# A three-layer attention and mixer kernel: the rounded copy of the keys is made by GpSimd instead of ScalarE

## The reference

```python
scores = scale * np.matmul(q, k.transpose(0, 1, 3, 2))
keep = is_sink | in_window            # keys 0..3, or 0 <= query - key < 128
scores = np.where(keep, scores, -1e9)
a = softmax(scores)
x = a @ v                             # then heads side by side: 768 x 512 per batch
# layer 2
h = relu(x @ w_in); u, v = h[..., :512], h[..., 512:]
v_n = (v - mean(v)) / sqrt(var(v) + 1e-6)
x = (u * (w_spatial @ v_n + b_spatial)) @ w_out
# layer 3
u = x + (relu(x^T @ w_tok1) @ w_tok2)^T
out = u + relu(u @ w_ch1) @ w_ch2
```

## Time and profile before

| | |
|---|---|
| median of 3 runs | 519.94 us (519.16 to 520.16) |
| profiled execution, its own time | 519.94 us |
| its span | 518.2 us |
| PE busy | 497.9 us (96%) |
| DVE busy | 214.0 us (41%) |
| ACT busy | 161.3 us (31%) |
| POOL busy | 161.2 us (31%) |

### The profile page before, as it was taken

The page is one execution under the profiler, slowest core; times in us unless marked ns, Lnnn a source line. Parts: engine busy times, 40 slices in busy tenths (PEclk is TensorE's granted clock), DMA queues, the critical chain, the costliest instruction groups (busy, mean ns, idle before and its releaser), DMA issues.

```text
span 518.2 us, 7223 instructions
## 1 busy us (share of the span) xinstructions
PE 497.9 (96%) x2712; PEld 442.6 (85%) x2712; DVE 214.0 (41%) x535; ACT 161.3 (31%) x337; POOL 161.2 (31%) x170
## 2 busy tenths in 40 slices
PE   1799999999999999999999999999999999999997
PEld 1698899999999989999888999888888888888885
DVE  4577777687567326755222233112121121211212
ACT  2466666577566332112211232101101001011010
POOL 5365535453332377801307903940000000000000
PEclk9999999999999999999999999999999999999999
DMA  7444233433320134300202410400011000010002
GB/s 263 127 144 140 90 100 103 135 102 104 103 64 1 54 117 135 99 0 1 76 1 78 128 39 20 140 24 2 0 43 39 0 1 0 31 52 1 0 1 81
DMA packets 19479, 34.19 MB, mean 66 GB/s; under 512 B 2288, under 2 KB 4848, under 8 KB 19440
## 3 DMA queue, kind: packets, MB, share of 16 engines
q1 hardware_dynamic: 19008, 33.55, 20.6%
q10 hardware_dynamic: 432, 0.13, 0.1%
HBM read 30.53 MB, written 3.15 MB: 65 GB/s over the span
## 4 chain that ended last, share of the span: by engine, by line
PE 92%; DVE 3%; issue 1%; DMA 1%; ACT 1%; DVEq 0%; ACTq 0%
PE bank L933 25%; PE bank L934 24%; PE bank L935 24%; PE bank L1006 7%; PE bank L972 3%; PE bank L948 3%; PE bank L949 2%; PE bank L1014 1%; DVE q_st L751 1%; PE bank L988 1%; DMA mask_scratch<-key 1%; PE bank L1166 1%; PE bank L1164 1%; DVE masked L760 1%; PE bank L980 0%
## 5 line engine op out<-in xcount | busy, mean ns | idle before, releaser
L922 DVE SCALAR_TENSOR_TENSOR hch_lo<-bank,hch_hi 128x512 fp32r<-128x512 f32 x36 | 24.9, 692 | 153.8 <-ACT hch_hi L696 153.8
L696 ACT ACTIVATE hch_hi<-bank 128x512 fp32r<-128x512 f32 x36 | 21.5, 598 | 169.0 <-PE bank L935 169.0
L586 ACT ACTIVATE probs<-masked,small 128x288 f32<-128x288 f32 (+1 forms) x96 | 48.9, 509 | 51.3 <-DVE small L760 50.8
L495 POOL TENSOR_TENSOR k_lo<-k_raw,k_hi 128x512 fp32r<-128x512 f32 x24 | 30.9, 1287 | 85.0 <-ACT k_hi L561 85.0
L760 DVE CUSTOM_DVE_ANT_0 masked<-bank,masks 128x288 f32<-128x288 f32 (+1 forms) x96 | 41.0, 427 | 36.9 <-PE bank L949 32.0
L935 PE MATMUL bank<-up_hi,wc_lo 128*128 128x512 f32 x144 | 56.0, 389 | 0.0
L934 PE MATMUL bank<-up_lo,wc_hi 128*128 128x512 f32 x144 | 56.0, 389 | 0.0
L933 PE MATMUL bank<-hch_hi,wc_hi 128*128 128x512 f32 x144 | 56.0, 389 | 0.0
L934 PE MATMUL bank<-hch_lo,wc_hi 128*128 128x512 f32 x144 | 56.0, 389 | 0.0
L933 PE MATMUL bank<-up_hi,wc_hi 128*128 128x512 f32 x144 | 56.0, 389 | 0.0
L935 PE MATMUL bank<-hch_hi,wc_lo 128*128 128x512 f32 x144 | 56.0, 389 | 0.0
(11 more groups left out here) (119 smaller groups left out, 1052.1 us busy)
## 6 DMA issues: line engine op xcount, KB each, us to landing
k_raw<-kT SPq DMA_DIRECT2D x24, 256.0 KB, 3.0
q_raw<-qT SPq DMA_DIRECT2D x24, 256.0 KB, 3.0
stage<-w_c SPq DMA_DIRECT2D x24, 256.0 KB, 2.7
v_sl<-vL SPq DMA_DIRECT2D x12, 264.0 KB, 3.1
outT<-out_sb SPq DMA_DIRECT2D x12, 256.0 KB, 2.1
stage<-w_sp SPq DMA_DIRECT2D x12, 192.0 KB, 2.6
stage<-w_in SPq DMA_DIRECT2D x8, 256.0 KB, 4.4
stage<-w_out SPq DMA_DIRECT2D x4, 256.0 KB, 3.0
```

What stands on the lines that cost most here:

```text
L495: pool.tensor_tensor(k_lo[:, hs, c0:c0 + P], raw, k_hi[:, hs, c0:c0 + P], ALU.subtract).then_inc(k_ready, 1)
L586: act.activation(probs[:, n % N_PROB, 0:w], masked[:, n % N_MASKED, 0:w], ACT.Exp, bias=least[:, n % 8:n % 8 + 1], scale=-1.0).then_inc(ex ...
L696: act.activation(hch_hi[:, u[2] % N_HCH, :], bank[:, :], ACT.Relu).then_inc(hi_ready, 1)
L922: dve.scalar_tensor_tensor(out=hch_lo[:, f % N_HCH, :], in0=bank[:, :], scalar=0.0, in1=hch_hi[:, f % N_HCH, :], op0=ALU.max, op1=ALU.subt ...
```

## The change

The rounding copy of the keys for groups 2 to 23 is removed from ACT and put on POOL, in front of the subtraction, with the same two waits. For groups 0 and 1 it stays on ACT. The function `k_high` is cut to those two groups, and the loop of ACT no longer calls it.

```diff
@@ gpsimd, k_prepare(g)
                 raw = k_raw[:, g % 2, :].rearrange("p (h c) -> p h c", c=P)
+                if g >= 2:
+                    pool.wait_ge(s_k[g % 2], 16 * (g // 2 + 1))
+                    if g >= 4:
+                        pool.wait_ge(scored, 4 * (g - 1))
+                    pool.tensor_scalar(k_hi[:, hs, c0:c0 + P], raw, 1.0, 1.0, ALU.mult, ALU.mult).then_inc(k_high_done, 1)
                 pool.wait_ge(k_high_done, g + 1)
                 pool.tensor_tensor(k_lo[:, hs, c0:c0 + P], raw, k_hi[:, hs, c0:c0 + P], ALU.subtract).then_inc(k_ready, 1)
@@ scalar, k_high(g)
-                t, half = divmod(g, 2)
-                c0 = 0 if t % 2 == 0 else P + SINKS
-                act.wait_ge(s_k[g % 2], 16 * (g // 2 + 1))
-                if g >= 4:
-                    act.wait_ge(scored, 4 * (g - 1))
-                act.activation(k_hi[:, 4 * half:4 * half + 4, c0:c0 + P], k_raw[:, g % 2, :].rearrange("p (h c) -> p h c", c=P),
+                half = g % 2
+                act.wait_ge(s_k[g % 2], 16)
+                act.activation(k_hi[:, 4 * half:4 * half + 4, 0:P], k_raw[:, g % 2, :].rearrange("p (h c) -> p h c", c=P),
                                ACT.Copy).then_inc(k_high_done, 1)
@@ scalar, loop over the steps
-                if n % 4 == 0 and 2 <= n // 4 + 1 < N_GROUP:
-                    k_high(n // 4 + 1)
```

## The result

The changed kernel takes 522.99 us (median of 6 runs, 521.07 to 524.14), the one before 519.75 us beside it (6 runs, 518.87 to 520.16). The ratio is 1.0063, with the interval 1.0042 to 1.0085: slower, by about as much as predicted. The profiled execution took 523.14 us, its span 521.4 us, 3.2 us more than before.

A forecast was written before the change was run, and what follows sets the result against it. Until about 59 us `q_low` on DVE repeatedly holds PE; then to 191 us PE alone bounds. The profiled 519.94 us plus 1.1 (start) plus 1.75 (groups 4, 6, 8) gives 522.8 us, range 519.5 to 524.3.

The forecast's parts named there:

- How `q_low` and POOL take turns: Shared port of DVE and POOL: `q_low` stands still until the running POOL operation ends, then needs 0.55 us.
- The one row on which I chose the side: At 99.58 us, POOL began 0.02 us ahead of `q_low` and went first; so POOL was assumed first.
- Step 1: Start: group 2's and 3's `k_lo` delay `q_low` of groups 1 and 2; costs 1.1 us, bounds 0 to 2.4.
- Step 2: Groups 4, 6 and 8: `k_lo` starts 0.02 us before `q_low`, delaying it 1.06, 0.61 and 0.08; sum 1.75 us.
- `q_low` first: Rival: `q_low` precedes `k_lo` at groups 4, 6, 8; group 8 gains 0.52 us, total 520.5; chance 0.25.
- Step 3: Later groups: `q_low` falls into `k_hi`, PE has slack 0.6; priced 0, upper end 1 us, including normalisation at line 803.
- my own signs: Trace signs of being wrong: those three `q_low` take 0.69, the chain meets `k_lo` itself, or the difference arises behind 60 us.
- hidden: Rival: whole kernel, everything hidden since the chain is PE alone for most of the span; 519.9 us, chance 0.12.
- paid back: Rival: at the start, a later start loses only half of step 1; 522.2 us, no separate chance given.
- Not slower: Rival: ACT's copy at 16.58 goes, neither early `q_low` is caught, group 8 gains 0.52; 519.0 us, chance 0.08.

The follow-up runs named there:

- experiment 7: Experiment 2 plus a tiny DVE memset right before `q_low` of groups 6 and 8; 521.19 us, ratio 1.0034 to the kernel before.
- experiment 10: The changed kernel with the copy on POOL only from group 3 on, group 2 staying on ACT; 519.95 us, ratio 0.9997 to the kernel before.
- experiment 3: The changed kernel with the copy on POOL for groups 2 and 3 only; 522.95 us, ratio 1.0072 to the kernel before.
- experiment 9: The changed kernel with SP's transfers from its loop turn 4 on held until DVE has masked group 2's first score; 521.74 us, ratio 1.0036.
- experiment 11: Experiment 2 plus two one-column DVE operations before `q_low` of groups 6 and 8; 520.79 us, ratio 1.0020 to the kernel before.
- experiment 6: Experiment 2 with the copy done twice on POOL from group 6 on; 518.48 us, ratio 0.9983 to the kernel before.
- experiment 2: The changed kernel with the copy on POOL only from group 4 on, groups 2 and 3 staying on ACT; 518.64 us, ratio 0.9985.
- experiment 1: The changed kernel with POOL's copy, from group 2 on, held until `q_low` of the group before is done; 519.92 us, ratio 1.0006.
- experiment 5: Experiment 2 with POOL's copy held until `q_low` of the group before is done; 518.07 us, ratio 0.9974 to the kernel before.
- experiment 12: Experiment 10 with POOL waiting, from group 4 on, for `q_low` of the group before; 517.17 us, ratio 0.9956 to the kernel before.
- experiment 8: Experiment 7's memsets plus experiment 5's wait for `q_low` from group 4 on; 518.06 us, ratio 0.9973 to the kernel before.
- experiment 4: The changed kernel with POOL held behind `q_low` before the keys of groups 5, 7 and 9 only; 521.89 us, ratio 1.0045.

## Why the prediction held, step by step

**How `q_low` and POOL take turns** held in every trace: in the first 170 us of all fourteen profiled executions, every `q_low` that took over 0.85 us ends 0.53 to 0.56 us behind the end of a POOL operation. The one row on which I chose the side has a lead of 0.02 us, and at that lead POOL won again (group 4 of the changed kernel). But at groups 6 and 8 the leads were 0.01 us or less, and there nothing follows from it: with 0.01 POOL won at 6 of experiment 7 and at 4 and 8 of experiment 10, and DVE at 8 of the changed kernel and of experiment 7. It is a tie.

**Step 1 was mis-sized: 1.1 us predicted, 2.5 measured at group 3, or 3.3 without the head start.** `q_low` of group 1 took the predicted 1.35. The mask subtraction of line 734 was caught (1.39 for 0.29, +1.10), which I had in the upper bound of 2.4 and not in the sum. That makes 1.8 us; with the head start of 0.8, which is luck, group 2 started 1.04 late. `q_low` of group 2 ended at 20.02 against my 20.15, but that is luck too: I had it in a `k_lo`, with over 1.4 us, and it came behind that `k_lo`, met a `win_hi` and took 0.93. After that two things that I had not foreseen: the three mask operations of line 708 in the chain at 20 us, held by a `win_lo`, 0.67 longer, and the gap, 0.80 longer. 1.04 + 0.67 + 0.80 = 2.51. Experiments 3 and 10 show that group 2's copy makes all of this, experiment 9 the gap's part of it.

**Step 2 was right at one group of three: 1.75 predicted, 1.23 measured.** Group 4 took 1.80 and cost 1.06 and a little. At 6 and 8 the rival came true: `q_low` first, 0.69, nothing lost. Where POOL does win there, my price holds: in experiment 11 groups 6 and 8 lose 0.76 us against the kernel before (groups 4 to 9), and I had 0.61 + 0.08.

**What `q_low` first is worth was priced too low: 0.52 in the rival, 1.04 measured.** The changed kernel gains 0.47 at group 7, 0.30 at 8 and 0.27 at 9. I had seen 8 only. At 7 PE before had waited for `p_cat` of ACT. The waits of PE (us in total, times, longest), before and after, 27 to 72 us:

```profile
PE bank L980 <- ACT p_cat L594: 0.6, 1, 0.6
```
```profile
PE bank L980 <- ACT p_cat L596: 0.2, 1, 0.2
```

ACT's lost copy isn't the reason, since before it stood behind that `p_cat`:

```profile
47.81 0.30 ACT L594 ACTIVATE p_cat<-probs 128x128 f32<-128x128 f32 x1
48.01 0.62 ACT L561 ACTIVATE k_hi<-k_raw 128x512 fp32r<-128x512 f32 x1
```

It is `q_low` of group 6, which leaves DVE 0.5 us earlier when it isn't caught; the masking behind it, the exponential and `p_cat` come earlier by as much. Three experiments show it: in 6, 7 and 11 ACT is as relieved as in experiment 2, but `q_low` of group 6 takes 1.15, 1.81 and 1.71, and their gain at group 7 is 0.0, where experiment 2, with 0.69, gains 0.5. So the prediction was right that ACT's copy stands on no path to PE there, and wrong in following `q_low` to the next score only.

**Step 3 was priced at 0 and cost 0.66 us.** `q_low` behaved as I worked out (about 0.98 at later even groups, with PE not waiting for it). The normalisation did not: behind the later `q_low`, line 803 started at 75.62 beside a `k_lo` and took 1.00 us, and PE then waited 0.42 us for the next `p_cat` of ACT. That lies inside my bound of 1 us, and experiments 1 and 5 lose nothing there.

**The sum came out right since the errors cancel.** Predicted +1.1 +1.75 +0 = +2.9. The trace: +2.51 +1.23 -1.07 +0.66 -0.1 = +3.2. The closeness is luck: the head start of 0.8 and the gains at groups 7 to 9 hide the start's true cost. By my own signs the account was half right: two of the three `q_low` took 0.69, which I had named as a sign of being wrong, and 0.66 us arose behind 60 us, where the chain was to be PE alone. The sign of the change is shown by experiments 2, 3 and 10: what is lost is lost through whom POOL meets, not through how long it works (experiment 6). The rivals "hidden" and "paid back" fall. "`q_low` first" was half true. "Not slower" needed the first catch to fail, and experiments 2, 5 and 12 are that case.

**What stays open.** Why one side wins a tie of 0.01 us in one execution and the other in the next; that this makes the wide scatter of the changed kernel (3.1 us) and of experiment 10 (3.4), against 1.5 in experiment 12, is argued and not shown. The first load has its part in such scatter (1.3 us between the profiled executions), and so has the moment at which PE changes its pace (up to 0.9 us, last section). Both also stand in the differences between experiments: of the 2.8 us by which experiment 12 is ahead of the kernel before at group 11, 0.6 is there at group 0 and 0.9 arises between groups 3 and 4, of which `q_low`'s 0.69 instead of 0.74 explains nothing. And the kernel before had caught `q_low` of its own (1.19 and 1.72 at groups 6 and 8). No run gives it the wait without moving the copy, so how much of the gain of experiments 5 and 12 is the wait alone isn't known.

## What to carry to other kernels

When work goes to an engine that takes turns with another, as POOL and DVE do here, don't add up its length; list who runs on the other engine at the moment it starts, above all short operations on the path to PE, and see who is first. Where both are released by the same event and arrive within 0.01 us, don't predict the winner but fix it with a wait: here the same move is +0.6% as it stands and -0.4% with one wait and without its first group. Follow a DVE operation that ends earlier or later beyond the matmul that waits for it: here it fed ACT, and ACT fed the next matmuls. And a start that is full of waits is its own case: what frees a buffer earlier also starts a transfer earlier, in front of something else.

## What was not expected of the hardware

- DVE operations with one input are held too. Line 803 takes 0.54 us alone and 1.00 at 75.62, where it ends 0.28 us behind `k_lo`; at 181.43 it ended 0.27 behind a POOL subtraction. The prediction had this for line 803 but not for the masks of line 708, which took 1.20 for 0.53, three together. The Trainium skill says that it can happen (SBUF — State Buffer, Who interferes with whom): `tensor_scalar` can enter a mode that uses both ports and then contends. The durations here agree; no run shows which mode these operations were in.
- The gap in the chain at 20 to 26 us was 2.86 us before, where the instruction packets went ahead of the data, 2.79 in experiment 9, where transfers were held back, and 3.66 in the changed kernel, where they went behind. That the wait for them makes the gap fits experiment 9; no run took the fetch itself away.
- PE works at half its later pace until about 30 us, though the granted clock reads 1.00 in both stretches. In experiment 12 the start to start distance of 288-column scores falls from 0.24 to 0.13 us between 27.6 and 30.4 us (about 288 columns at 1.2 GHz and at 2.4), and eight matmuls of one kind take 1.00 us:

```profile
27.57 0.44 PE L955 MATMUL bank<-k_hi,q_st 128*128 128x288 f32 x1
27.81 0.44 PE L956 MATMUL bank<-k_lo,q_st 128*128 128x288 f32 x1
...
28.76 1.00 PE L1013 MATMUL bank<-v_sl,p_t 128*128 128x66 f32 x8
...
30.30 0.29 PE L955 MATMUL bank<-k_hi,q_st 128*128 128x288 f32 x1
30.43 0.29 PE L956 MATMUL bank<-k_lo,q_st 128*128 128x288 f32 x1
```

In the kernel before the eight took 1.74 us, at about the same place:

```profile
29.55 1.74 PE L1006 MATMUL bank<-v_sl,p_t 128*128 128x66 f32 x8
```

From the first score of group 3 to the transposes of x (line 988) PE takes 3.5 to 3.6 us in the two kernels and in experiments 2, 3, 7, 10 and 11, 3.4 in 1, 2.8 to 3.1 in 5, 6, 8 and 9, and 2.7 in 4 and 12. I have no run that says what sets the moment of the change.
